# Attention and two gated networks on one core: queries, keys and values handed over in the layout the multiplications use

## What is computed

```python
k_sum = k.reshape(B, H, nb, 32, D).max(axis=3)      # 24 block keys: maxima over 32 keys
v_sum = v.reshape(B, H, nb, 32, D).mean(axis=3)     # 24 block values: means
scores_l = where(|i - j| < 16, scale * q @ k.T, -1e9)
scores_s = scale * q @ k_sum.T + log(32)
a = softmax(concat([scores_l, scores_s]))
x = a @ concat([v, v_sum])                          # then heads side by side: 1536 x 512
h = relu(x @ w_in); conv = 3 taps over tokens; x = (h * sigmoid(conv)) @ w_out
xn = layer_norm(x) * g_ln
out = x + relu(xn @ w_ch1) @ w_ch2
```

## Time and profile before

| | |
|---|---|
| median of three runs | 462.5 us (461.82 to 463.79) |
| span of the profiled execution | 460.9 us |
| TensorE busy | 452.0 us (98%), 3114 multiplications |
| VectorE, ScalarE, GpSimd busy | 275.0, 200.1, 268.3 us |
| DMA | 35.28 MB, 74725 packets, 57632 of them under 512 bytes |
| granted TensorE clock | 1.000 (full speed) over the span |

### The profile page before, as it was taken

The page is one execution under the profiler, slowest core; times in us unless marked ns, Lnnn a source line. Parts: engine busy times, 40 slices in busy tenths (PEclk is TensorE's granted clock), DMA queues, the critical chain, the costliest instruction groups (busy, mean ns, idle before and its releaser), DMA issues.

```text
span 460.9 us, 8619 instructions
## 1 busy us (share of the span) xinstructions
PE 452.0 (98%) x3114; PEld 400.5 (87%) x3114; DVE 275.0 (60%) x630; ACT 200.1 (43%) x503; POOL 268.3 (58%) x405
## 2 busy tenths in 40 slices
PE   7899999999999999999999999999999999999997
PEld 6687888989989889989889988998998899889885
DVE  4999976876666967974674254546762244124333
ACT  3898997433335746436243143422421233123210
POOL 2559689999945000097898889750042687878000
PEclk9999999999999999999999999999999999999999
DMA  9998951212102000002115324120020211220003
GB/s 229 213 232 197 195 140 53 92 47 91 47 0 93 0 1 0 1 0 91 54 41 143 109 93 93 67 91 1 26 89 23 93 46 47 91 93 0 1 0 137
DMA packets 74725, 35.28 MB, mean 77 GB/s; under 512 B 57632, under 2 KB 68924, under 8 KB 74684
## 3 DMA queue, kind: packets, MB, share of 16 engines
q1 hardware_dynamic: 71164, 33.85, 27.1%
q10 hardware_dynamic: 3520, 0.88, 0.9%
HBM read 28.83 MB, written 3.15 MB: 69 GB/s over the span
## 4 chain that ended last, share of the span: by engine, by line
PE 96%; DMA 1%; DVE 1%; issue 1%; ACT 1%; ACTq 0%; DVEq 0%
PE two L1689 10%; PE two L1687 10%; PE two L1688 10%; PE two L1664 9%; PE two L1667 8%; PE two L1666 8%; PE two L1460 5%; PE two L1462 5%; PE two L1461 5%; PE two L1595 5%; PE two L1596 5%; PE two L1594 5%; PE two L1413 3%; PE two L1445 3%; PE two L1424 3%; PE two L1342 3%
## 5 line engine op out<-in xcount | busy, mean ns | idle before, releaser
L640 POOL TENSOR_TENSOR asum<-wst 128x256 f32<-128x256 f32 x26 | 21.8, 838 | 93.4 <-PE two L1462 50.2
L1664 PE MATMUL two<-combo,wa 128*128 128x384 f32 x224 | 75.8, 338 | 0.0
L1667 PE MATMUL two<-combo,wa 128*128 128x384 f32 x224 | 75.6, 337 | 0.0
L1666 PE MATMUL two<-combo,wa 128*128 128x384 f32 x224 | 75.2, 336 | 0.0
L1689 PE MATMUL two<-wv,h 128*128 128x512 f32 x192 | 75.0, 391 | 0.0
L1687 PE MATMUL two<-wv,h 128*128 128x512 f32 x192 | 74.8, 390 | 0.2 <-DVE h L946 0.2
L1688 PE MATMUL two<-wv,h 128*128 128x512 f32 x192 | 75.0, 390 | 0.0
L1023 DVE TENSOR_TENSOR u<-two,u 128x384 f32<-128x384 f32 x16 | 8.9, 558 | 90.2 <-PE two L1667 90.2
L1267 ACT ACTIVATE h<-u 128x384 fp32r<-128x384 f32 x16 | 8.4, 525 | 122.4 <-DVE u L1023 122.4
L574 POOL TENSOR_SCALAR pn<-ex,rinv 128x120 f32<-128x120 f32 x96 | 34.8, 383 | 19.1 <-DVE rinv L736 18.4
L634 POOL TENSOR_TENSOR wa<-asum,wa 128x256 fp32r<-128x256 f32 x52 | 43.2, 831 | 4.3
(11 more groups left out here) (119 smaller groups left out, 981.0 us busy)
## 6 DMA issues: line engine op xcount, KB each, us to landing
wst<-in_moe_w_ch SPq DMA_DIRECT2D x26, 512.0 KB, 3.2
vW<-in_v SPq DMA_DIRECT2D x13, 288.0 KB
kn<-in_k SPq DMA_DIRECT2D x15, 192.0 KB, 3.8
qn<-in_q SPq DMA_DIRECT2D x15, 192.0 KB, 3.7
out<-y SPq DMA_DIRECT2D x11, 256.0 KB, 2.0
wst<-in_moe_w_in SPq DMA_DIRECT2D x8, 256.0 KB, 3.1
wst<-in_moe_w_out SPq DMA_DIRECT2D x8, 256.0 KB, 2.8
tok<-xq SPq DMA_DIRECT2D x32, 48.0 KB, 2.0
```

Of the source, the lines that this page charges most:

```text
L1664: nc.tensor.matmul(o, wk[:, 0, kk], ck[:, 0, kk], start=(first and kk == 0), stop=False, skip_group_check=True)
L1666: nc.tensor.matmul(o, wk[:, 0, kk], ck[:, 1, kk], start=False, stop=False, skip_group_check=True)
L1667: ins = nc.tensor.matmul(o, wk[:, 1, kk], ck[:, 0, kk], start=False, stop=(kk == 1), skip_group_check=True)
```

## The change

`kernel()` lays q, k and v out on the host side of the call: q and k by pairs with the head dimension first (128 x 768 for each pair), v by pairs with tokens first (768 x 128), k and v with 16 zeros ahead and behind. `conv_w` and `g_ln` are handed over with partitions first. On the chip this removes, for each pair, the 12 transposes (L1342), the three window copies (L699, for the first pair L705 and L1053) and the query copy (L1045); it removes the first warming transposes between the first queries and the first scores, the turn of the vectors (L1550), and the zeroing of window edges. Keys now come as overlapping windows straight into `kW`, one DMA of 128 x 12 runs of 384 bytes for a pair; queries come straight into `qT` (3072-byte runs); values come by one DMA of 96 x 12 runs of 512 bytes. `kW` and `qT` have three buffers. Block maxima are read from the windows in SBUF. The freed PSUM goes to a second bank for the turned probabilities and to the block means. The first pair's keys come in three DMAs of four blocks, their maxima are taken in three parts, and VectorE itself writes the block keys of the first four blocks. All hand-written orders are written anew.

```diff
+        def k_windows(p, b0, nb):
+            a = k[p, :, 0:1]
+            return bass.AP(a.tensor, a.offset + QB * b0, [[SP, P], [QB, nb], [1, KEYS]])
+        def v_windows(p):
+            a = v[p, 0:1]
+            return bass.AP(a.tensor, a.offset, [[P, KEYS], [QB * P, NQ], [1, P]])
+        def probs_at(n):
+            return bank[6] if n < LATE and n % 2 else bank[2]
             def load_k(p):
-                if p >= 2:
-                    sp.wait_ge(ktr_ready, p - 1)
-                b, hp = p // PPB, p % PPB
-                for h in range(2):
-                    sp.dma_start(kn[:, p % 2, :, h],
-                                 k[b, 2 * hp + h].rearrange("(t p) d -> p t d", p=P)).then_inc(kn_in[p % 2], 16)
+                if p >= 3:
+                    sp.wait_ge(s_ready, GPP * (p - 2))
+                sp.dma_start(kW[p % 3][:, :, 0:KEYS], k_windows(p, 0, NQ)).then_inc(k_in[p % 3], 16)
+            def first_k():
+                for g in range(GPP):
+                    sp.dma_start(kW[0][:, GB * g:GB * (g + 1), 0:KEYS], k_windows(0, GB * g, GB)).then_inc(k_first_part(g), 16)
+            first_k()
             load_k(1)
             load_q(1)
-            sp.wait_ge(pool_init, 1)
-            for dst, src in v_parts(0)[2:4]:
-                sp.dma_start(dst, src).then_inc(v_in[0], 16)
+            load_v(0)
+            load_v(1)
             load_k(2)
...
             def key_max(p):
-                dve.wait_ge(ktr_ready, p + 1)
-                if p >= 1:
-                    dve.wait_ge(ksb_done, p)
-                nc.vector.tensor_reduce(out=ks[:], in_=ps_kq[:, TOK0:TOK0 + S].rearrange("p (n i) -> p n i", i=BLK),
-                                        op=ALU.max, axis=AX.X).then_inc(ks_done, 1)
+                dve.wait_ge(k_in[p % 3], chunk_in(p))
+                dve.wait_ge(ksb_done, p)
+                block_maxima(p, 0, NQ)
...
             pe.wait_ge(pool_link, IDENT_LINKS)
             warm(13)
-            keys_t(0)
-            queries_t(0)
-            warm(4)
             scores(0)
-            keys_t(1)
             scores(1)
-            queries_t(1)
             scores(2)
             block_means(0)
-            keys_t(2)
             scores(3)
             probs_t(0)
             scores(4)
-            block_means(1)
-            scores(5)
             probs_t(1)
-            queries_t(2)
+            scores(5)
+            probs_t(2)
             outputs(0)
...
+            outputs(17)
             hidden(0, [0, 1])
             scores(21)
-            hidden(0, [2, 3])
             probs_t(18)
+            hidden(0, [2, 3, 4])
             scores(22)
-            outputs(17)
+            hidden(0, [5])
             block_means(7)
             probs_t(19)
+            hidden(0, [6, 7])
             scores(23)
             outputs(18)
...
```

More of the change, by code:

```diff
@@ L222, in conv_gated_attention_kernel, with chunk_in, k_first_part @@
         w1_cols = w_ch1.rearrange("(c p) f -> p c f", p=P)
+        def chunk_in(p):
+            return 16 * (p // 3 + 1)
+        def k_first_part(g):
+            return k_first[g] if g < GPP - 1 else k_in[0]
         def v_windows_in(p):
-            return 16 * (sum(len(v_parts(o)) + 2 for o in range(p % 3, p, 3)) + len(v_parts(p)))
+            return 16 * (3 * (p // 3) + 1)
         def v_loads(p):
-            return v_windows_in(p) + 16 * 2
-        TOK0 = P
+            return 16 * 3 * (p // 3 + 1)
         def block_of(n, j):
@@ L506, in _ @@
             load_vsum(7)
-            for n in range(3, 8):
-                load_w(n)
+            load_w(3)
+            load_w(4)
+            load_w(5)
+            load_w(6)
+            load_w(7)
             for l in range(NLOAD):
@@ L852, in _ @@
             score_max(18)
-            key_max(7)
-            window_keys(7)
             row_sums(17)
@@ L1071, in probs_out @@
                     act.wait_ge(o_ready, n - 1)
-                nc.scalar.copy(pts[0:KW, n % 2], ps_pt[0:KW]).then_inc(pts_done, 1)
+                nc.scalar.copy(pts[0:KW, n % 2], probs_at(n)[0:KW]).then_inc(pts_done, 1)
             def x_high(n):
@@ L1338, in _ @@
         def _(pe):
-            def transposes(src, dst, done):
-                for t in range(T):
-                    ins = nc.tensor.transpose(dst[:, TOK0 + P * t:TOK0 + P * (t + 1)],
-                                              src[:, t].rearrange("p h d -> p (h d)"), ident[:])
-                ins.then_inc(done, 1)
             def warm(count):
                 for i in range(count):
-                    nc.tensor.transpose(ps_o[2][:, 0:P], ident[:], ident[:])
+                    nc.tensor.transpose(ps_h[0][:, 0:P], ident[:], ident[:])
             def block_means(p):
@@ L1513, in _ @@
             outputs(7)
+            outputs(8)
+            scores(13)
             probs_t(9)
-            outputs(8)
             block_means(4)
+            scores(14)
             probs_t(10)
-            scores(13)
-            queries_t(5)
-            scores(14)
-            keys_t(6)
+            probs_t(11)
             outputs(9)
-            probs_t(11)
             scores(15)
+            probs_t(12)
             outputs(10)
-            probs_t(12)
             outputs(11)
             scores(16)
+            block_means(5)
@@ L1529, in _ @@
             probs_t(13)
-            queries_t(6)
-            block_means(5)
             scores(17)
+            probs_t(14)
             outputs(12)
-            probs_t(14)
+            probs_t(15)
+            scores(18)
             outputs(13)
-            scores(18)
-            keys_t(7)
-            probs_t(15)
-            outputs(14)
             block_means(6)
             scores(19)
+            outputs(14)
+            outputs(15)
             probs_t(16)
-            queries_t(7)
@@ L1544, in _ @@
-            outputs(15)
+            probs_t(17)
+            scores(20)
             outputs(16)
-            pe.wait_ge(consts_in, 32)
-            pe.wait_ge(q_done, NPAIR)
-            nc.tensor.transpose(ps_kq[:, 0:KD + 3 * KF], rows[:],
-                                ident[0:KD + 3 * KF, 0:KD + 3 * KF]).then_inc(cols_ready, 1)
-            scores(20)
-            probs_t(17)
-            pe.wait_ge(w_done, w_ready("in", 0))
-            pe.wait_ge(cols_done, 1)
-            pe.wait_ge(x_done, GPP * PPB)
+            outputs(17)
@@ L1572, in _ @@
             probs_t(21)
-            hidden(1, range(KD))
+            hidden(1, [3, 4])
             outputs(20)
-            hidden(1, range(KD, 2 * KD))
+            outputs(21)
             probs_t(22)
-            outputs(21)
+            hidden(1, [5, 6])
             probs_t(23)
+            hidden(1, [7])
             outputs(22)
```

452 lines of the change are left out of this document (197 added, 255 removed).

## The result

The kernel became slower, by 1.3%. It takes 468.5 us (median of 4 runs, 467.51 to 472.04) against 462.9 for the kernel before, measured beside it: a ratio of 1.0132, 95% interval 1.0093 to 1.0172. The forecast was 454.1. The profiled execution spans 466.5 us, 5.6 more than before. A few executions take far longer than the rest of the same kernel (2514 us for one of the kernel before), and the medians and ratios in this document leave them out.

The account below looks back on a forecast made before the run. TensorE was busy 452.0 of 460.9 us, with ScalarE and VectorE also full in the steady stretch; ScalarE would become the bound. Attention ends 8.8 us earlier, less 0.4 for weights: 460.9 - 8.4 + 1.6 = 454.1 us, range 449.5 to 457.8.

Parts of the forecast that it names:

- Start: Up to the first scores: keys all there at about 6.0 us, first scores at 6.8 instead of 8.37, 1.6 us won.
- Ramp: First scores to exps of group 4: exps(0) at 8.6, then 8.1 us instead of 11.1, so exps(4) at 16.7.
- rival B: TensorE runs slow through the ramp, costing 3.2 us: about 457.5 us; chance 0.13 together with Rival D's far end.
- Steady: Exps of group 4 to group 18, 14 groups: ScalarE sets the pace, 32.0 us (30.5 to 34.5) instead of 35.6.
- Rival C: DMA becomes the bound once its rate is below 226 GB/s; at 200, 467 us, slower than before; chance 0.04.
- The rule weighed: For key loads: line rate needs runs of at least 512 bytes; 384-byte runs at 284 GB/s put first scores at 7.5 us.
- Tail: Exps of group 18 to the third step of `hidden`: 22.7 us (21.8 to 24.5) instead of 23.4.
- Weights: GpSimd's weight splits before `project(0)`: between 1.5 us of slack left and 1.5 lacking, 0.4 us charged.
- Rival D: Weights come late by 1 to 3 us more than charged: 455 to 457 us; far end shares 0.13 with rival B.
- Behind it: The block behind attention, from the third step of `hidden` to the end: unchanged at 380.7 us.
- Key maxima from SBUF: VectorE's key maxima, read from SBUF instead of PSUM: the same 0.96 us (0.7 to 1.2).
- Rival A: TensorE stays the bound and all its removed work, 13 us, is won: 449.5 us; chance 0.12.

Follow-up runs that it names:

- e_alone: Changed kernel with each form of load moved by itself behind the last store: key windows 295 to 218 GB/s, value windows 295 to 204, queries up to 403.
- e_warm: Changed kernel with TensorE kept busy by extra transposes in the ramp and before the two stalls: 467.4 us, ratio 1.0077.
- e_light2: Changed kernel, but from pair 3 on each load of keys, queries and values brings only the first of 12 blocks: 458.0 us, ratio 0.9892.
- e_half: Changed kernel, but from pair 3 on loads bring half the columns of each key and value window, in as many packets: 459.8 us, ratio 0.991.
- e_alone3: Window loads in 512-byte runs by themselves behind the last store, on different numbers of partitions: 128 held 347 GB/s, 96 fell from 289 to 172.
- e_order: Changed kernel with only SyncE's list reordered, loads put ahead of spreads that wait: 466.9 us, ratio 1.0075.
- e_novs: Changed kernel, but from pair 3 on the spread of block values writes only one of 12 blocks: 464.9 us, ratio 1.004.
- e_v128: Changed kernel with value windows loaded on 128 partitions instead of 96, a third more value bytes: 466.1 us, ratio 1.0064.
- e_best: e_stage plus more warming transposes, four weight quarters split earlier on GpSimd, and the value loads of e_v128: 459.4 us, ratio 0.9926.
- e_stage: e_order with keys from pair 1 on loaded once as 3200-byte rows and laid out in windows by a VectorE copy: 462.75 us, ratio 0.998.
- e_alone2: Value-window loads by themselves behind the last store, with other distances between runs: first four groups started at 265 to 326 GB/s and fell to about 200.

## Why the prediction was wrong

Of the 14.4 us between 454.1 and 468.5, in the order of its sum:

*Start.* First scores at 6.81 us, 6.8 forecast; the keys landed at 6.06, 6.0 forecast. DMA moved 306 GB/s from 2.2 to 6.1 us, and key windows alone at 295 to 274 in e_alone, so the estimated 320 was a little high. Right.

*Ramp.* exps(0) at 9.01 instead of 8.6, exps(4) at 18.27 instead of 16.7: 1.6 us short. The first scores took 1.08 us, not 0.64, and e_warm got 1.1 us back with transposes alone. This is rival B, at a third to a half of its price of 3.2 us; I had weighed it as a rival and put nothing of it into the sum. The last 0.5 us have no run of their own.

*Steady.* 42.6 us instead of 32.0: 10.6 us, three quarters of the error, and **the step that failed is "at 320 GB/s and over it takes 5.4 us of a pair's 6.9 and is hidden by three buffers"**. The working on the engines was right: e_light2 has exps(4) to exps(18) in 50.75 - 18.62 = 32.1 us. With half the bytes of keys and values e_half took 8.7 us off. The rate was 224 GB/s instead of 320, so a pair's 1.72 MB took 7.7 us instead of 5.4, against a pair's 6.9 us of engine work. Buffers don't hide that: three of them cover a late transfer, not a queue that is too slow for as long as the stretch lasts.

By itself 7.7 us a pair gives 36 us for 14 groups, not 42.6. The rest shows when the bytes are counted from the start, length times rate by stretch: until exps(18) DMA moved 13.6 MB in 60.8 us (223 GB/s), in the kernel before 12.2 MB in 56.8 us (216 GB/s). The new kernel comes to exps(4) 3.0 us sooner, with 4.0 MB moved instead of 4.8, and needs more bytes in all. A queue that is full nearly from the start doesn't let the gain of start and ramp be kept; the steady stretch pays for it. That is my reading of the rows; e_warm, which came to exps(4) earlier and to `project(0)` no earlier, agrees with it.

The evidence lay in a row that I had quoted. In the earlier trace rows the steady stretch of before has a DMA share of 0.99 at 210 GB/s. I read the 210 as what was asked for, and took the capacity from the earlier trace rows. After e_half and e_light2 the better reading is that the queue had little left to give: a fourth resource about as full as TensorE, VectorE and ScalarE. For the kernel before this is argued: no run slowed DMA there, and from 21 to 57 us no wait of an engine in its trace names a DMA, so the queue kept up. The share isn't exact either, it reads 1.20 in places. The subtraction that I did for three engines should have had a fourth line: 0.99 x 35.6 = 35.2 us of DMA, and the change adds 13% to its bytes, 39.8 us, the largest of the four. Put in place of the 32.0 that gives 462 us, about as before. The measured stretch moved 9.5 MB where this line has 8.4 (39.8 us at 210 GB/s), the loads that start and ramp no longer covered. What the low clock adds on top was not separated.

*Rival C* named the mechanism: DMA as the bound, from 226 GB/s down, 467 us. That its 467 lies near 468.5 is partly luck. It reckoned with 200 GB/s; at the measured 224 its own sum gives 7.7 us a pair against 7.6, under 1 us of loss in six pairs, and it had nothing for the gain at the front being paid back. It had 0.04, against it stood "284 GB/s were held for 7 us with shorter runs", and that argument doesn't carry: a rate is that of a form of load, and two forms of this list, 512-byte runs on 96 partitions and spreads on twelve, had no row of their own.

*The rule weighed.* By the Trainium skill, "DMA: Bandwidth & Descriptors", section Specifications, runs under 512 bytes lose line rate. The keys (384 bytes) moved at 295 to 274 GB/s, under the 327 to 328 of 512-byte rows on as many partitions, so e_alone agrees in the direction. But the values have 512-byte runs and were the slowest load at 204 to 242 GB/s. The measurement decides: length of the run didn't rank these loads, e_alone3 shows the same run at 347 and at 172.

*Tail.* 82.79 - 60.84 = 21.95 us, 22.7 forecast. Right within 0.8, on the good side.

*Weights.* 2.2 us of wait for L568 where 0.4 was charged and 1.5 the bound. It is 2.2 us in e_order, e_half, e_warm, e_novs, e_v128 and e_light2 too, whether `project(0)` comes at 78.9 or at 89.4: it is the order of GpSimd's list and not DMA. Five splits (7 to 11) stand behind `normalise(23)`, and they took 80.34 to 89.29 us, 1.8 us each, where the forecast had 7.8 us for all five. e_best, with four of them there, has no such wait at `project(0)`, but by the times above it lost as much ahead of it. Rival D's mechanism is right, then, and comes on top of whichever case holds; as a rival with a chance of its own it was in the wrong place, it was a term of the sum with too narrow bounds.

*Behind it.* 0.6 us more than in the kernel before; in e_light2 2.0, as its granted clock stood at 0.53 for 3.6 us after the wait (1.2 GHz is 0.50; 9 matmuls in the row above, 18 in as long a stretch of e_best).

*Key maxima from SBUF* took 0.95 us, 0.96 forecast. *Rival A* needs TensorE to be the bound; in e_light2, where DMA is out of the way, it is busy 29.6 of the 32.2 us of the steady stretch and ScalarE is the fuller one, so A falls.

Two slips of the working changed nothing: "9 us go from the steady stretch on two engines" should read 7.7 and 6.9 by its own lines, and SyncE's list has three DMAs fewer a pair, not four.

In sum: start 0, ramp 1.6, steady 10.6, tail -0.8, weights 2.0 (with what lies between the third `hidden` and `project(0)`), behind it 0.6. That is 14.0 us, the whole difference of the profiled span (466.5) from the forecast one (454.1 - 1.6 = 452.5). The last 0.4 of the 14.4 are the median against the profiled span.

What stays open: why the mixed list ran at 224 GB/s, under what most of its forms reach alone; e_v128 shows that the form of the values is a part of it. For e_best the late weights and VectorE's nine waits are in its trace, but no run takes one of them away. The effects of the runs (e_v128 2.4, e_stage over e_order 4.1, spreads 3.6, order 1.6) overlap and are not to be added.

## What to carry to other kernels

When a change takes work from the full engines, do the same subtraction for the DMA queue: share times length of the stretch is its busy time now, and the change's bytes scale it. A DMA share near 1.0 is a warning whatever the GB/s beside it: here the kernel before still kept up at 0.99 and 210 GB/s, and with 13% more bytes the new one did not. The share by itself proves no bound; a run with half the bytes does. The rate to plan with is that of the same stretch and the same form of load, not the best one in the trace. Count the bytes from the start of the program, since a full queue takes back what is won ahead of it. If a layout by DMA replaces transposes, count the bytes that overlapping windows carry twice, and give every new form of load (how many partitions, how long the runs) a measurement of its own first.

## What the hardware showed that was not expected

- Loads of 512-byte runs on 128 partitions, 9 on each, held 347 GB/s; runs of the same length on 96 partitions, 12 on each, started at 265 to 326 and fell to 172 to 221, on 64 to 190, on 112 to 238 (e_alone2, e_alone3). Writing a third more bytes to fill all 128 was faster in the kernel, 254 GB/s against 224 at the same DMA share of 0.98 (e_v128, 2.4 us). Why the rate falls within a few us was not tried.
- Copies within the chip onto twelve partitions moved 82 to 97 GB/s (e_alone).
- The granted clock fell to about half after TensorE had waited 3.2 and 3.7 us, and in e_light2 after 2.21 us, but not behind the 2.2 us in the changed kernel. Transposes in the ramp and in front of the stalls were worth 1.1 us in all by the medians (e_warm). The 1.00 in the first 7 us doesn't fit the durations: 13 transposes took 3.04 us there, 0.23 each, and six took 0.85, 0.14 each, at 9.51 us.
